# Windowed attention ahead of an expert layer: value matmuls with V as the loaded operand, x turned back together with the gate weights, row sums on ScalarE

## The chip, the cores and the metric
One Trainium2 chip, one NeuronCore. The metric is the device time of one execution in microseconds (us), as the median of several executions. Engines: PE is TensorE (PEld its weight loads), DVE is VectorE, ACT is ScalarE, POOL is GpSimd, SP is SyncE, which here only issues DMAs ("SPq").

## The reference
Three layers follow each other, in float32.

```
scores = (q @ k.T) / sqrt(64); keep keys 0..3 (sinks) and the last 128 up to the query
a = softmax(scores);  x = a @ v                     # 2 batches x 8 heads, 768 x 64
x -> (1536, 512);  logits = x @ w_gate + log1p(exp(x @ w_noise)) * noise
top-2 of 8 experts;  x = sum_k weight_k * relu(x @ w1[e_k]) @ w2[e_k]
h = x @ w_in;  out = (h * tanh(softplus(h))) @ w_out
```

## The kernel before, in words
The program is one core's, with every engine's order of work written out by hand and semaphores between them. Four stages follow: attention (to about 123 us), routing (to about 143 us), 31 expert slots of 128 rows, and the last layer.

**Attention.** The 16 heads make 8 head pairs. A head pair has 6 query tiles of 128 rows, so there are 48 tiles ("units" u). The loops of PE, ACT and DVE take two tiles at a time, 24 double steps, of which the middle ones run in a hardware loop (`stream_loop`). A query tile sees its own 128 keys, the 128 keys before and 4 sink keys. For one tile:

- PE `scores` (L1172): 2 heads x 3 split-precision matmuls, 64 rows each, up to 264 columns, into one of two pairs of PSUM banks. It waits until the exponentials of tile u-2 are done.
- DVE `merge_step` (L841): a predicated copy puts the previous tile's masked scores over the own tile's, then L860 takes the row minimum (the scores are negated) for the exponent's bias. The first tile of a head pair masks against a constant; the second also hides the sinks twice seen.
- ACT `exp_step` (L653): one exponential for each head into `probs` (2 buffers).
- PE `turn_probs` (L1199): two transposes of 128 x 128 and one of 8 sink columns. ACT `pT_step` (L662) copies them to SBUF, the sinks by an instruction of their own (L668).
- POOL `cut_probs` (L539): two selects separate the probabilities of own and previous keys.
- PE `values` (L1217): the probabilities are the loaded operand (128 columns) and V streams, 130 columns for own and previous keys, 162 for the sinks. A float32 matmul is two passes, each a weight load and a stream. V carries a column of ones, so the sum of the row comes out beside the product, and 16 columns of V times the gate and noise weights, so the logits come out too.
- DVE `norm_step` (L870): the reciprocal of the sum, then one multiply from PSUM into `x_sb`.

V times the gate weights is made by PE `gate_parts` (L1186) from a turned copy of V (`v_turn`, 404.5 KB a head pair): three steps of two tiles each, in the later tiles of the head pair before, copied next to V by ACT `gate_step` (L670).

q and k of the next head pair are rounded by ACT (`round_qk`, L648, four pieces: two in the first double step of a head pair, two in the second) and their remainders taken by DVE (`qk_remainder`, L862). The first of these waits for both loads.

**SP's queue** sets when things are loaded and stored (L432). For head pairs i from 2 to 7, in order:

```
sp.wait_ge(qk_ready, 4 * (i - 1)); load_qk(i)
sp.wait_ge(gates_made, ...);       load_turned(i)
sp.wait_ge(pv_ready, QT * (i - 1)); load_v(i)
store_x(i - 2)       # first: sp.wait_ge(x_ready, QT * (i - 1))
two 512 KB blocks of the first expert's weights (i = 2 to 5)
if i == 4: seven 256 KB stores that fill y_dram
```

POOL's `first_set` (L526) rounds and splits those blocks in the second half of the attention stage, from tile 14 on. After the last tile, DVE `gate_sums` (L894) adds the 8 parts of each logit; the routing follows from there.

Of the kernel before, what the change touches and what calls it, by code (L numbers as in the profile page):

```python
# [4 lines left out]
P = 128  # L5
# [9 lines left out]
def stream_loop(eng, count, body):  # L15

    body(0)
    with eng.Fori(1, count - 1) as i:
        body(i)
    body(count - 1)  # L20


# [11 lines left out]
def attention_moe_mish(nc, shape, q, k, v, v_sinks, v_turned, noise, w1, w2, w_in, w_out, out, n_sink, window):  # L34
# [4 lines left out]
    i32 = mybir.dt.int32  # L39
# [20 lines left out]
    VW = D + 1 + GL  # L60
    SEC = P + NS
    SK = 2 * NS + 1
# [47 lines left out]
    v_in = [attn.tensor(f"v_in{i}", [P, QT, 2, VW], fp32) for i in range(2)]  # L110
    v_sink = [attn.tensor(f"v_sink{i}", [P, 2, VW], fp32) for i in range(2)]
    VT_GATE, VT_TILES, VT_SINK = 0, 2 * GL, 2 * GL + S
    WIDE = 2 * (D + 1)
    v_turn = attn.tensor("v_turn", [P, S + SK + 2 * GL], fp32)
    qT = [attn.tensor(f"qT{i}", [P, 2, S], f32r) for i in range(2)]
    kT = [attn.tensor(f"kT{i}", [P, 2, QT * SEC], f32r) for i in range(2)]
    probs = [attn.tensor(f"probs{i}", [P, 2 * SEC], fp32) for i in range(2)]
    pT = [attn.tensor(f"pT{i}", [P, 2, P], fp32) for i in range(2)]
    pT_own = [attn.tensor(f"pT_own{i}", [P, 2, P], fp32) for i in range(3)]
    pT_prev = [attn.tensor(f"pT_prev{i}", [P, 2, P], fp32) for i in range(3)]  # L120
    pT_sink = [attn.tensor(f"pT_sink{i}", [P, P], fp32) for i in range(3)]
# [8 lines left out]
    x_sb = route.tensor("x_sb", [P, QT, NP, 2, VW], fp32)  # L130
    later = route.tensor("later", [P, P], fp32)
# [9 lines left out]
    ramp_i = route.tensor("ramp_i", [P, P], i32)  # L141
    rt = {}
    for name, cols in (("nb", 4), ("rc", 4), ("seg", E * QT), ("seg_e", E * QT), ("noise", E * NT), ("lgs", GL * NT),
                       ("enx", E * NT), ("sp", E * NT), ("lg", E * NT), ("eq", E * QT), ("cum", E * QT), ("cut", E * QT),
                       ("oh", 2 * E * NT), ("m1", NT), ("m2", NT), ("gap", NT), ("s1", NT), ("c", E * NT), ("inc", E * NT),
                       ("pos", E * NT), ("up", E), ("ns", E), ("incn", E), ("excn", E), ("sel", 2 * E * NT),
                       ("p01", 2 * NT), ("den", NT), ("tab", 32 * E), ("ex", 32)):
        rt[name] = route.tensor("rt_" + name, [P, cols], fp32)
    tok_i = route.tensor("tok_i", [P, 2 * NT], i32)
# [78 lines left out]
    with ctx:  # L228
# [11 lines left out]
        v_turn_loaded = sem("v_turn_loaded")  # L240
# [26 lines left out]
        pT_sink_ready = sem("pT_sink_ready")  # L267
        WEIGHTS_FROM = 14
        pT_cut = sem("pT_cut")
        pv_ready = sem("pv_ready")  # L270
        x_ready = sem("x_ready")
        dve_step = sem("dve_step")
        units_begun = sem("units_begun")

        gates_made = sem("gates_made")
        gates_ready = sem("gates_ready")
# [68 lines left out]
        OB = [bank[6], bank[7]]  # L345
        OUT_HEAD = 256

        def out_heads(b):

            return OB[b].rearrange("p (h d) -> p h d", h=2)[:, :, 0:VW]  # L350

# [17 lines left out]
        GATE_TILES = 2  # L369
        GATE_STEPS = QT // GATE_TILES  # L370
        GATE_AT = QT - GATE_STEPS
        GATE_FIRST = [TP[1][:, n * P:(n + 1) * P] for n in range(GATE_STEPS)]
        GATE_OUT = [TP[0][:, 3 * P:4 * P], TP[1][:, 3 * P:4 * P]]
# [6 lines left out]
        def at_unit(it, n):  # L380

            return it + n // QT // 2, n // QT % 2, n % QT

        MERGES = [0]
        for t in range(QT):
            MERGES.append(MERGES[t] + 1 + (t == 1) + (t > 0 and window < P))
        PER_PAIR = MERGES[QT]

# [13 lines left out]
        def _(sp):  # L402
# [4 lines left out]
            def load_v(i, par):  # L407
                if i < 2:
                    sp.wait_ge(sinks_cleared, i + 1)
                sp.dma_start(v_in[par][:, :, :, 0:D + 1], v[i]).then_inc(v_loaded[par], 16)  # L410
                sp.dma_start(v_sink[par][0:SK, :, 0:D + 1], v_sinks[i]).then_inc(v_loaded[par], 16)

            def load_turned(i):
                sp.dma_start(v_turn[:], v_turned[i]).then_inc(v_turn_loaded, 16)
# [9 lines left out]
            load_turned(0)  # L424
# [3 lines left out]
            sp.wait_ge(gates_made, GATE_STEPS)  # L428
            load_turned(1)
            sp.dma_start(rt["noise"][:].rearrange("p (j e) -> p j e", j=NT), noise.rearrange("(j p) e -> p j e", p=P)).then_inc(route_in_loaded, 16)  # L430
            assert UNITS <= 2 * (NP - 2)
            for i in range(2, NP):  # L432
                sp.wait_ge(qk_ready, 4 * (i - 1))
                load_qk(i, i % 2)
                sp.wait_ge(gates_made, GATE_STEPS * i)
                load_turned(i)
# [8 lines left out]
                if i == 4:  # L445
# [31 lines left out]
        def _(pool):  # L477
# [17 lines left out]
            for i in range(3):  # L495
                nc.gpsimd.memset(pT_sink[i][:], 1.0)
# [15 lines left out]
            nc.gpsimd.iota(ramp_i[:], pattern=[[1, P]], base=0, channel_multiplier=0)  # L512
# [8 lines left out]
            nc.gpsimd.tensor_copy(ramp[:], ramp_i[:])  # L521
# [17 lines left out]
            def cut_probs(u):  # L539
                b = u % 3  # L540
                pool.wait_ge(pT_ready, u + 1)
                wait(pool, pv_ready, u - 2)
                ins = nc.gpsimd.affine_select(out=pT_own[b][:], in_=pT[u % 2][:], compare_op=ALU.is_ge, fill=0.0, base=0,  # L543
                                              pattern=[[0, 2], [1, P]], channel_multiplier=-1)
                if u % QT > 0:
                    ins = nc.gpsimd.affine_select(out=pT_prev[b][:], in_=pT[u % 2][:], compare_op=ALU.is_ge, fill=0.0, base=-1,
# [3 lines left out]
            for n in range(0, NP * QT, 2):  # L550
                cut_probs(n)
                cut_probs(n + 1)
# [90 lines left out]
        def _(act):  # L643
# [9 lines left out]
            def exp_step(hp, par, t):  # L653
                u, b = QT * (2 * hp + par) + t, t % 2
                act.wait_ge(bias_ready, u + 1)
                wait(act, probs_transposed, u - 1)
                for hd in range(2):
                    ins = nc.scalar.activation(probs[b][:, hd * SEC:(hd + 1) * SEC], SC[b][:, hd, SEC:2 * SEC], ACT.Exp,  # L658
                                               bias=rt["nb"][:, 2 * b + hd:2 * b + hd + 1], scale=-1.0)
                ins.then_inc(probs_ready, 1)  # L660

            def pT_step(hp, par, t):  # L662
                u, b = QT * (2 * hp + par) + t, t % 2
                act.wait_ge(probs_transposed, u + 1)
                wait(act, pT_cut, u - 1)
                nc.scalar.activation(pT[b][:], TP[b][:, 0:2 * P].rearrange("p (h q) -> p h q", h=2), ACT.Copy).then_inc(pT_ready, 1)  # L666
                wait(act, pv_ready, u - 2)
                nc.scalar.activation(pT_sink[t % 3][0:2 * NS, :], TP[b][0:2 * NS, 2 * P:3 * P], ACT.Copy).then_inc(pT_sink_ready, 1)  # L668

            def gate_step(hp, par, step, src):  # L670
                i = 2 * hp + par
                act.wait_ge(gates_made, GATE_STEPS if isinstance(hp, int) and i == 0 else GATE_STEPS * i + step + 1)
                if step == 0:
                    wait(act, pv_ready, QT * (i - 1))
                at = slice(GATE_TILES * step, GATE_TILES * (step + 1))
                ins = nc.scalar.activation(v_in[par][:, at, :, D + 1:VW],
                                           src[:, 0:GATE_TILES * 2 * GL].rearrange("p (t h e) -> p t h e", t=GATE_TILES, h=2), ACT.Copy)
                if step == GATE_STEPS - 1:
# [801 lines left out]
```

## Time and profile before

| What | us |
|---|---|
| median of 3 runs (lowest, highest) | 805.99 (805.07, 806.14) |
| the profiled execution, its own time | 804.93 |
| its span on the core | 803.2 |
| PE, PEld, DVE, ACT, POOL busy | 775.8, 643.2, 517.0, 278.8, 304.0 |

In the profile times count from the start of the span. A busy time of PE is not PE at its peak, since the ends of matmuls are modelled and overlap; the distance between the starts of two instructions tells the pace. A row of the timeline gives start, duration, engine, line, operation, output and inputs, shape, how many instructions were merged into it and, in brackets, how long the engine was idle before it and for whom.

### The profile page before, as it was taken

The numbers are of one execution on the slowest core, as the hardware profiler recorded it, in microseconds if no ns is written. First come the engines' busy times: TensorE is split into PE (matmuls) and PEld (weight loads), VectorE is DVE, ScalarE is ACT, GpSimd is POOL, SyncE is SP. The second block draws the span as 40 slices with busy tenths as digits, with TensorE's granted clock in tenths as the row PEclk, the third lists the DMA queues.
The fourth block names the chain that finished last, engine by engine and source line by source line (L and its number), as shares of the span: only waits on it lengthen the run. The fifth ranks groups of instructions, "written<-read, shape, count | busy, mean of one in ns | idle before, by whom it ended". The sixth has DMA issues, their size and how long they took to land.

```text
span 803.2 us, 13152 instructions
## 1 busy us (share of the span) xinstructions
PE 775.8 (97%) x4116; PEld 643.2 (80%) x4117; DVE 517.0 (64%) x944; ACT 278.8 (35%) x553; POOL 304.0 (38%) x307
## 2 busy tenths in 40 slices
PE   9999994999999999999999999998999999999997
PEld 6888883788888888888888888786888888888886
DVE  5686876454454454454544544558998888888776
ACT  5665652203110302003030300145555555454453
POOL 3366672929281652817337554550111010000000
PEclk9999996999999999999999999999999999999999
DMA  7689562736372451715427353120100100000001
GB/s 204 184 237 304 146 207 55 208 103 199 104 223 79 125 175 37 228 62 156 144 62 227 102 184 109 37 66 1 53 27 27 53 27 27 1 28 25 1 0 53
DMA packets 61442, 86.15 MB, mean 107 GB/s; under 512 B 30104, under 2 KB 34200, under 8 KB 61400
## 3 DMA queue, kind: packets, MB, share of 16 engines
q1 hardware_dynamic: 43400, 37.23, 15.1%
q10 hardware_dynamic: 13600, 33.96, 14.1%
q0 software_dynamic: 4400, 14.42, 6.4%
q8 instruction: 23, 0.38, 0.2%
q14 instruction: 19, 0.16, 0.1%
HBM read 69.35 MB, written 16.25 MB: 107 GB/s over the span
## 4 chain that ended last, share of the span: by engine, by line
PE 88%; DVE 5%; ACT 2%; SPq 1%; issue 1%; DMA 1%; another core or an unknown queue 1%; POOL 0%; DVEq 0%; ACTq 0%; POOLq 0%
PE bank L1321 21%; PE bank L1332 21%; PE bank L1393 15%; PE bank L1374 15%; PE bank L1229 4%; PE bank L1305 3%; PE bank L1182 2%; PE bank L1298 2%; PE bank L1192 1%; PE bank L1214 1%; PE bank L1232 1%; SPq L448 1%; PE bank L1167 1%; DMA k_in<-in_k 1%
## 5 line engine op out<-in xcount | busy, mean ns | idle before, releaser
L563 POOL TENSOR_TENSOR wgt<-stage,wgt 128x1024 f32 (+1 forms) x64 | 151.2, 2403 | 106.6 <-ACT wgt L738 106.6
L1332 PE MATMUL bank<-wgt,hT 128*128 (+1 forms) x744 | 185.7, 398 | 0.0
L1321 PE MATMUL bank<-wgt,xT 128*128 (+1 forms) x744 | 182.4, 394 | 1.5 <-DVE xT L1049 1.5
L1321 PEld LDWEIGHTS bank<-wgt,xT 128*128 128x128 f32 x744 | 137.3, 188 | 28.9 <-DVE xT L1049 1.7
L1332 PEld LDWEIGHTS bank<-wgt,hT 128*128 128x128 f32 x744 | 135.2, 188 | 25.8
L738 ACT ACTIVATE wgt<-stage 128x1024 f32 (+1 forms) x64 | 61.6, 1045 | 269.6 <-PE bank L1332 259.4
L1393 PE MATMUL bank<-wgt,gT 128*128 128x512 f32 x576 | 141.2, 395 | 4.9 <-DVE gT L1110 4.9
L1374 PE MATMUL bank<-x2T,wgt 128*128 128x512 f32 (+1 forms) x588 | 138.1, 385 | 0.9 <-DVE x2T L1087 0.9
L1393 PEld LDWEIGHTS bank<-wgt,gT 128*128 128x128 f32 x576 | 108.5, 190 | 28.6 <-DVE gT L1110 6.1
L1374 PEld LDWEIGHTS bank<-x2T,wgt 128*128 128x128 f32 x588 | 108.7, 188 | 23.0 <-POOL wgt L635 1.1
L1055 DVE TENSOR_SCALAR h<-bank 128x512 f32<-128x512 f32 x62 | 42.9, 691 | 63.9 <-PE bank L1321 61.8
L1059 DVE CAST hT<-bank 128x512 fp32r<-128x512 f32 x62 | 42.9, 692 | 58.3 <-PE bank L1305 58.3
L808 ACT ACTIVATE recd<-nume,ones 128x512 f32<-128x512 f32 x48 | 34.8, 725 | 90.8 <-DVE nume L1133 90.8
L1070 DVE COPY y_sb<-bank 128x512 f32<-128x512 f32 x31 | 21.4, 692 | 69.5 <-PE bank L1332 55.9
L609 POOL DMA_INDIRECT ya<-y_dram,y_idx x10 | 10.2, 1019 | 132.0 <-PE bank L1366 114.9
L1061 DVE TENSOR_TENSOR hT<-bank,hT 128x512 fp32r<-128x512 f32 x62 | 42.9, 692 | 2.1
L1124 DVE TENSOR_SCALAR expv<-expv 128x512 f32<-128x512 f32 x48 | 20.7, 431 | 32.4 <-ACT expv L802 32.4
L795 ACT ACTIVATE gT<-nume 128x512 fp32r<-128x512 f32 x48 | 30.3, 632 | 28.0 <-DVE nume L1101 27.7
L543 POOL TENSOR_SCALAR_AFFINE_SELECT pT_own<-pT 128x256 f32<-128x256 f32 x48 | 20.9, 436 | 48.6 <-ACT pT L666 48.1
L1305 PEld LDWEIGHTS bank<-ident,h 128*128 128x128 f32 x248 | 30.6, 140 | 9.5 <-DVE h L1055 1.6
L1305 PE MATMUL bank<-ident,h 128*128 128x128 f32 x248 | 37.3, 273 | 0.5 <-DVE h L1055 0.4
L658 ACT ACTIVATE probs<-bank,rt_nb 128x132 f32<-128x132 f32 x96 | 30.1, 366 | 21.8 <-DVE rt_nb L860 21.6
(169 smaller groups left out, 963.7 us busy)
## 6 DMA issues: line engine op xcount, KB each, us to landing
stage<-in_moe_w ACTq DMA_DIRECT2D x48, 512.0 KB, 4.3
stage<-in_moe_w SPq DMA_DIRECT2D x16, 512.0 KB, 6.7
y_dram<-y_sb SPq DMA_DIRECT2D x31, 256.0 KB, 2.4
stage<-in_moe_w_in ACTq DMA_DIRECT2D x8, 512.0 KB, 4.5
stage<-in_moe_w_out ACTq DMA_DIRECT2D x8, 512.0 KB, 3.7
v_turn<-in_v_turned SPq DMA_DIRECT2D x8, 404.5 KB, 3.7
v_in<-in_v SPq DMA_DIRECT2D x8, 390.0 KB
x_dram<-x_sb SPq DMA_DIRECT2D x16, 192.0 KB, 3.2
```

Of the source, the lines that this page charges most:

```text
L563: nc.gpsimd.tensor_tensor(cols(parity, 1, u * UNIT, UNIT), stage[:, u, :], cols(parity, 0, u * UNIT, UNIT).bitcast(fp32), ALU.subtract).th ...
L738: nc.scalar.activation(cols(parity, 0, u * UNIT, UNIT), stage[:, u, :], ACT.Copy).then_inc(rounded, 1)
L808: nc.scalar.activation(recd[p][:], nume[p][:], ACT.Ln, bias=ones1[:, 1:2]).then_inc(ln_ready, 1)
L1055: V.tensor_scalar(h[:, half * 512:(half + 1) * 512], bank[half][:], 0.0, None, ALU.max).then_inc(h_ready, 1)
L1059: V.tensor_copy(hT[:, 0, 4 * half:4 * half + 4], src).then_inc(hT_rounded, 1)
L1061: V.tensor_tensor(hT[:, 1, 4 * half:4 * half + 4], src, hT[:, 0, 4 * half:4 * half + 4].bitcast(fp32), ALU.subtract).then_inc(hT_ready, 1)
L1229: T.matmul(OB[b][:, to:to + WIDE], (pT_prev if back else pT_own)[t % 3][:, hd, :], v_in[par][:, t - back].rearrange("p h d -> p (h d)")[:, ...
L1305: ins = T.transpose(bank[3 + half][:, n * P:(n + 1) * P], h[:, c * P:(c + 1) * P], ident[:])
L1321: ins = T.matmul(HA[half][:], xT[:, a, c, :], cols(par, b, c * F + half * 512, 512), start=c == 0 and n == 0, stop=c == NC - 1 and n == 2)
L1332: ins = T.matmul(YB[kk % 2][:], hT[:, a, c, :], cols(par, b, NC * UNIT + c * DM, DM), start=c == 0 and n == 0, stop=c == F // P - 1 and n ...
L1374: ins = T.matmul(hid_bank(fg)[:, tok], wgt[:, 0, b, c * F2 + f * P:c * F2 + (f + 1) * P], x2T[g % 2][:, a, c, tok], start=c == 0 and n == ...
L1393: ins = T.matmul(bank[s][:], gT[fg % 2][:, a, s * P:(s + 1) * P], wgt[:, 1, b, f * DM:(f + 1) * DM], start=f == 0 and n == 0, stop=f == NF ...
```

## The change
The value matmul is turned round: halves of V (128 keys x 64 columns, one for each head) are loaded and the turned probabilities stream, so that x comes out turned, head 0 in output partitions 0 to 63 and head 1 in 64 to 127. ACT copies it to SBUF (`copy_xT`), and a matmul with `turn_back` (an identity beside the gate weights) gives x with its logit parts. The sinks go through the same copies as the other keys. The row sums come from the exponentials' accumulator output; POOL adds 1e-9 and DVE takes one reciprocal for two tiles. Row minima, x copy and norm are one instruction for two tiles. `probs`, `pT`, `pT_own` and `pT_prev` have 4 buffers. The steps of a tile are spread over more double steps: scores in step u, turned in u+2, values in u+4, turned back and normed in u+6. `v_turn`, `gate_parts` and `gate_step` go. The loops are unrolled. The fill of y_dram moves from i == 4 to i == 7. The diff's core:

```diff
-                sp.dma_start(v_in[par][:, :, :, 0:D + 1], v[i]).then_inc(v_loaded[par], 16)
+                sp.dma_start(v_in[par][:], v[i]).then_inc(v_loaded[par], 16)
...
             for i in range(2, NP):
                 sp.wait_ge(qk_ready, 4 * (i - 1))
                 load_qk(i, i % 2)
-                sp.wait_ge(gates_made, GATE_STEPS * i)
-                load_turned(i)
                 sp.wait_ge(pv_ready, QT * (i - 1))
                 load_v(i, i % 2)
                 store_x(i - 2)
...
-                if i == 4:
+                if i == NP - 1:
                     sp.wait_ge(consts_ready, 1)
...
+            def pad_sums(u):
+                nc.gpsimd.tensor_scalar(scale_cols("rs", u, 2), scale_cols("rs", u, 2), 1.0e-9, 1.0, ALU.add,
+                                        ALU.mult).then_inc(sums_padded, 2)
+            for n in range(0, PROBS + 2, 2):
+                if n > 0:
+                    cut_probs(n - 2)
+                    cut_probs(n - 1)
+                    pad_sums(n - 2)
...
+            def exp_step(u):
+                b, m = u % 2, u % 4
                 act.wait_ge(bias_ready, u + 1)
+                wait(act, probs_transposed, u - 3)
                 for hd in range(2):
+                    ins = nc.scalar.activation(probs[m][:, hd * SEC:(hd + 1) * SEC], SC[b][:, hd, SEC:2 * SEC], ACT.Exp,
+                                               bias=rt["nb"][:, 2 * b + hd:2 * b + hd + 1], scale=-1.0,
+                                               accum_out=scale_cols("rs", u, 1)[:, hd:hd + 1])
                 ins.then_inc(probs_ready, 1)
+            def pT_step(u):
                 act.wait_ge(probs_transposed, u + 1)
+                wait(act, pv_ready, u - 3)
+                nc.scalar.activation(pT[u % 4][:], TP[u % 2][:, 0:3 * P].rearrange("p (h q) -> p h q", h=3), ACT.Copy).then_inc(pT_ready, 1)
+            def copy_xT(u, count):
+                to = xT_att[u // 2 % 2]
+                act.wait_ge(pv_ready, u + count)
+                wait(act, x_turned, u // 2 * 2 - 2)
+                nc.scalar.activation(to[:, u % 2:u % 2 + count], turned_out(u, count), ACT.Copy).then_inc(xT_copied, count)
...
+            for u in range(0, PROBS, 2):
+                i, t = at_unit(u)
+                if u > 0:
+                    pT_step(u - 2)
+                    pT_step(u - 1)
+                exp_step(u)
+                exp_step(u + 1)
+                if u >= 4:
+                    copy_xT(u - 4, 2)
+                if i + 1 < NP and t < 4:
+                    par1 = (i + 1) % 2
+                    if t == 0:
+                        wait(act, scores_ready, QT * i)
+                        act.wait_ge(q_loaded[par1], 16 * ((i + 1) // 2 + par1))
+                        act.wait_ge(k_loaded[par1], 16 * ((i + 1) // 2 + par1))
+                    round_qk(par1, t)
+                    round_qk(par1, t + 1)
...
+            def row_minima(u, count):
+                b = u % 2
+                dve.wait_ge(merged, merges[0])
+                V.tensor_reduce(rt["nb"][:, 2 * b:2 * (b + count)], banks[:, 2 * b:2 * (b + count), SEC:2 * SEC], AX.X,
+                                ALU.min).then_inc(bias_ready, count)
+            def norm_step(u, count):
+                i, t = at_unit(u)
+                dve.wait_ge(scales_ready, u + count)
+                dve.wait_ge(x_turned, u + count)
+                scales = scale_cols("rs", u, count).rearrange("p (b h) -> p b h", h=2).unsqueeze(3)
+                V.tensor_tensor(x_sb[:, t:t + count, i], back_out(u, count), scales.broadcast_to([P, count, 2, VW]),
+                                ALU.mult).then_inc(x_ready, count)
...
+            for u in range(0, PROBS, 2):
+                i, t = at_unit(u)
+                merge(u)
...
+                merge(u + 1)
...
+                    row_minima(u, 2)
+                if u >= 4:
+                    row_scales(u - 4)
+                if t > 0 and i + 1 < NP:
+                    qk_remainder(i + 1, t - 2)
+                    qk_remainder(i + 1, t - 1)
+                if u >= 6:
+                    norm_step(u - 6, 2)
...
+            def values(u):
+                i, t = at_unit(u)
+                par, m, to = i % 2, u % 4, turned_out(u, 1)[:, 0]
...
+                wait(pe, xT_copied, u // 2 * 2)
                 pe.wait_ge(pT_cut, u + 1)
+                parts = [(v_in[par][:, t], pT_own[m][:, 0], pT_own[m][:, 1])]
+                if t > 0:
+                    parts.append((v_in[par][:, t - 1], pT_prev[m][:, 0], pT_prev[m][:, 1]))
+                parts.append((v_sink[par], pT[m][:, 2], pT[m][:, 2]))
+                for n, (keys, *of) in enumerate(parts):
                     for hd in range(2):
+                        ins = T.matmul(to[hd * D:(hd + 1) * D], keys[:, hd], of[hd], start=n == 0, stop=n == len(parts) - 1)
+                ins.then_inc(pv_ready, 1)
+            def turn_x_back(u):
...
+                pe.wait_ge(xT_copied, u + 1)
+                wait(pe, x_ready, u // 2 * 2)
+                T.matmul(back_out(u, 1)[:, 0], xT_att[u // 2 % 2][:, u % 2], turn_back[:, u // QT % PPB], start=True, stop=True).then_inc(x_turned, 1)
+            for u in range(0, PROBS, 2):
+                scores(u)
+                scores(u + 1)
+                if u == 0:
+                    fill(2)
+                else:
+                    turn_probs(u - 2)
+                    turn_probs(u - 1)
+                if u == 2:
+                    fill(1)
+                if u >= 6:
+                    turn_x_back(u - 6)
+                    turn_x_back(u - 5)
+                if u >= 4:
+                    values(u - 4)
+                    values(u - 3)
+            turn_probs(PROBS - 2)
+            turn_probs(PROBS - 1)
+            for u in (PROBS - 6, PROBS - 4):
+                turn_x_back(u)
+                turn_x_back(u + 1)
+                values(u + 2)
+                values(u + 3)
+            turn_x_back(PROBS - 2)
+            turn_x_back(PROBS - 1)
```

## Rows read from the trace of the kernel before

**Rows 1.** Timeline of PE in the attention stage: starts of the score blocks, two tiles each.

```profile
6.11 0.97 PE L1182 MATMUL bank<-kT,qT 64*128 64x132 f32 x12
...
34.34 0.97 PE L1182 MATMUL bank<-kT,qT 64*128 64x132 f32 x12
...
38.45 1.00 PE L1182 MATMUL bank<-kT,qT 64*128 64x264 f32 x12
...
42.69 0.99 PE L1182 MATMUL bank<-kT,qT 64*128 64x264 f32 x12
...
48.00 0.97 PE L1182 MATMUL bank<-kT,qT 64*128 64x132 f32 x12
...
113.77 0.99 PE L1182 MATMUL bank<-kT,qT 64*128 64x264 f32 x12
```

**Rows 2.** Timeline of PE, the rest of the double step that starts at 38.45.

```profile
39.38 0.71 PE L1229 MATMUL bank<-v_in,pT_own 128*128 128x130 f32 x4
39.93 0.44 PE L1232 MATMUL bank<-v_sink,pT_sink 128*128 128x162 f32 x2
40.20 0.61 PE L1229 MATMUL bank<-v_in,pT_own 128*128 128x130 f32 x4
...
41.09 0.44 PE L1232 MATMUL bank<-v_sink,pT_sink 128*128 128x162 f32 x2
41.37 0.38 PE L1214 MATMUL bank<-ident,probs 128*128 128x128 f32 x2
41.59 0.27 PE L1215 MATMUL bank<-ident,probs 128*8 128x128 f32 x1
```

**Rows 3.** Timeline of DVE at the end of the stage: the two gate sums.

```profile
121.07 1.24 DVE L898 TENSOR_REDUCE rt_lgs<-x_sb 128x80 f32<-128x640 f32 x1
...
122.78 0.37 DVE L898 TENSOR_REDUCE rt_lgs<-x_sb 128x16 f32<-128x128 f32 x1
```

**Rows 4.** Timeline of DVE in the double step of 38.45.

```profile
39.26 0.43 DVE L850 COPY_PREDICATED bank<-later,bank 128x256 f32<-128x256 uint32 x1 [0.73 <-PE bank L1182]
...
40.52 0.43 DVE L860 TENSOR_REDUCE rt_nb<-bank 128x2 f32<-128x264 f32 x1
...
41.42 0.55 DVE L868 SCALAR_TENSOR_TENSOR qT<-q_in,qT 128x384 fp32r<-128x384 f32 x1
...
42.19 0.33 DVE L878 TENSOR_TENSOR x_sb<-bank,rt_rc 128x162 f32 x1
```

**Rows 5.** ACT: timeline of the same step, then its shortest group by form.

```profile
40.19 0.63 ACT L658 ACTIVATE probs<-bank,rt_nb 128x132 f32<-128x132 f32 x2 [0.19 <-DVE rt_nb L860]
...
41.90 0.39 ACT L666 ACTIVATE pT<-bank 128x256 f32<-128x256 f32 x1 [0.28 <-PE bank L1215]
...
L679 ACT ACTIVATE v_sink<-bank 9x32 f32<-9x32 f32 x8 | 1.4, 172 | 0.0
```

**Rows 6.** Timeline of SP's queue: one pass with expert blocks, the y fill, one without.

```profile
25.77 1.04 SPq L420 DMA_DIRECT2D x_dram<-x_sb  x2
...
28.88 0.43 SPq L405 DMA_DIRECT2D k_in<-in_k  x1
...
55.63 7.68 SPq L448 DMA_DIRECT2D y_dram<-ident  x7
...
82.50 1.04 SPq L420 DMA_DIRECT2D x_dram<-x_sb  x2
...
84.22 0.55 SPq L405 DMA_DIRECT2D k_in<-in_k  x1
```

**Rows 7.** The k loads' time from issue to landing, and ACT's wait after the y fill.

```profile
DMA to landing us min/median/max: 4.5/5.9/7.3
...
69.09 0.52 ACT L650 ACTIVATE qT<-q_in 128x384 fp32r<-128x384 f32 x1 [2.14 <-DMA k_in<-in_k]
```

**Rows 8.** PE gap and clock: busy PE, PEld, DVE, ACT, POOL by stretch, PEclk, DMA share, GB/s.

```profile
543.60:547.80 4.20, 0.35 (x2) 0.00 (x0) 2.62 (x5) 2.46 (x4) 0.00 (x0) 1.00 0.01 2
547.90:551.30 3.40, 3.40 (x8) 2.74 (x9) 3.31 (x5) 2.60 (x5) 0.00 (x0) 0.50 0.00 0
```

More of the change, by code:

```diff
@@ L378, in of_group, with at_unit @@
             return rt[name][:, g * IN_GROUP:(g + 1) * IN_GROUP]
[L380 to L387, printed above, removed]
+        def at_unit(u):
+            return u // QT, u % QT
         FIRST = 3
@@ L839, in heads, with merge @@
                 return a.unsqueeze(1).broadcast_to([P, 2, a.shape[1]])
-            def merge_step(hp, par, t):
-                u, b = QT * (2 * hp + par) + t, t % 2
+            merges = [0]
+            def merge(u):
+                b, t = u % 2, u % QT
                 dve.wait_ge(scores_ready, u + 1)
@@ L870, in norm_step @@
[L870 to L879 removed]
+                    merges[0] += 1
@@ L1232, in values @@
-                T.matmul(out_heads(b), pT_sink[t % 3][:], v_sink[par][:],
-                         start=False, stop=True).then_inc(pv_ready, 1)
-            def body(it):
-                last = isinstance(it, int) and it == NP // 2 - 1
-                first = isinstance(it, int) and it == 0
-                for n in range(0, 2 * QT, 2):
-                    hp, par, t = at_unit(it, n)
-                    final = last and n == 2 * QT - 2
-                    scores(hp, par, t)
-                    scores(hp, par, t + 1)
-                    if first and n == 0:
-                        for step in range(GATE_STEPS):
-                            gate_parts(0, step, GATE_FIRST[step])
-                    else:
-                        if first and n == 2:
-                            fill(1)
-                        values(*at_unit(it, n - 2))
-                        if not final:
-                            values(*at_unit(it, n - 1))
-                    turn_probs(hp, par, t)
-                    if first and n == 0:
-                        fill(1)
-                    if final:
-                        values(*at_unit(it, n - 1))
-                    turn_probs(hp, par, t + 1)
@@ L1448 @@
     vt = inputs["v"].reshape(pairs, 2, tiles, P, dim)
[L1449 to L1452 removed]
+    laid["v"] = vt.transpose(0, 3, 2, 1, 4)
+    held = _np.zeros((pairs, 2 * sinks, 2, dim), _np.float32)
     for h in range(2):
[L1454 to L1467 removed]
+        held[:, h * sinks:(h + 1) * sinks, h] = vt[:, h, 0, 0:sinks]
     laid["v_sinks"] = held
+    both = _np.concatenate([inputs["moe_w_gate"], inputs["moe_w_noise"]], axis=1)
+    laid["gates"] = both.reshape(heads // 2, 2 * dim, -1).transpose(1, 0, 2)
     arrays, args = {}, []
```

345 lines of the change are left out of this document (114 added, 231 removed).

## The prediction, made before the changed kernel ran

> **What bounds the kernel now.** I read four views in this order: the starts of the score matmuls, which mark the steps of the attention stage; one step on each engine; SP's own queue; the clock. The attention stage takes 24 double steps, each two query tiles of one head pair; call them D0 to D23, so that head pair i has D(3i), D(3i+1) and D(3i+2). They start at 6.11, ..., 34.34 (D6), 38.45 (D7), 42.69 (D8), 48.00 (D9), ..., 113.77 (D23) [rows 1]. One double step is 4.11 us without gate matmuls; the third of a head pair, with two sets of them, is 5.31; a head pair is 13.66. The steps are full of TensorE work: in D7 the score block takes 0.93 (38.45 to 39.38), the value matmuls 0.45 per four and 0.28 per two sink passes (40.20 to 41.09 to 41.37), a turn of probabilities 0.11 an instruction (two in 0.22) [rows 2]. Sum: 0.93 + 2 x (0.89 + 0.28) + 2 x 0.33 + about 0.2 = 4.1, which is the step. So TensorE bounds this stage. A change of matmul shape costs about 0.1 on each side of the first instruction: the first four value passes take 0.55, the later ones 0.45 [rows 2]; with the gap before them I count 0.2 per change of shape, two changes per double step.
>
> All after the routing (the expert and Mish stages) is untouched by the diff, so the question is when the gate sums of the last tile are ready: 122.78 + 0.37 = 123.15 now [rows 3].
>
> **The change, part by part.**
>
> TensorE. Value matmuls: 8 value and 4 sink passes per tile (12, where 10 were), each with 64 weight columns, the two heads to different halves of the output partitions. A pass streams 128 columns, as the 130 of now, so 0.11 each [rows 2]. In sequence that is 1.31 per tile; with the two heads side by side 0.66. No row shows column halves. What rows show is the nearest case, the scores, where the heads take different row halves: 12 passes of up to 264 columns in a block of 0.93 including both changes of shape, against 12 x 0.11 = 1.3 in sequence [rows 2]. I take 0.66, the row it resembles most, and keep 1.31 as the other end. The page "TensorEngine Tiling (Array Packing)" of the Trainium skill, section "Key Properties", says that tiles work independently and in parallel, and also that a change of tiling mode drains the engine; by the first the sum stays as I have it, by the second alone it gains one more change of shape per double step, which the next sentence counts from rows anyway. Double step: scores 0.72 (0.93 less 0.2), turns 0.66, turning x back 4 passes of 160 columns, the 0.14 of the 162-column sink passes [rows 2], 0.55, values 1.32, three changes of shape 0.6: 3.85 (3.6 where one of the two tiles is the first of its sequence). The gate matmuls go.
>
> The new chain inside a step. Both tiles now share one row-minimum instruction, after both merges. From the start: the merge begins at +0.81 (39.26), 0.43; the second ends at +1.65; the reduction of 528 columns: 0.43 for 264 [rows 4] plus 264 x about 1.04 ns = 0.71, to +2.4; four exponentials, two take 0.63 with a pitch of 0.27 [rows 5]. The row sums add an accumulator read after each. No row has it: below 0, above 0.17, the smallest ScalarE instruction [rows 5]; I take 0.1, since short instructions overlap here. The last exponential ends at +4.05, and the second tile's scores of the next step may start 0.36 after the first's: a step of 3.7 to 3.85, in the first step of a head pair 4.05 (longer merge, sink merge). So TensorE and this chain tie near 3.9, against 13.66 / 3 = 4.55 now. VectorE: 2.0 for merges, minima and reciprocal, at most 1.1 for two remainders (0.55 each), 0.5 for the norm (0.33 for 162 columns, 320 now) [rows 4]. ScalarE: two wider copies 0.8 (0.39 for 256 columns [rows 5]), exponentials 1.5, copy of x 0.3, rounding 0.9: 3.5. POOL: four cuts of 0.41 and up to 1.8 of weight rounding, 3.5, and has a step of slack. All just below 3.9. The gate copies and the sink copy on ScalarE go; they were hidden by TensorE, so worth nothing alone.
>
> SP's queue, where I expect the change to be decided. SP does for each i: load q, k of head pair i; wait for the values of pair i-2; load v; **wait for x of pair i-2**, store it; load two expert blocks (i = 2 to 5); then load q, k of i+1. Now x of pair i-2 is normalised in D(3i-3); k is issued 3.1 after the store (25.77 to 28.88) [rows 6], lands 4.5 / 5.9 / 7.3 (lowest, median, highest) later [rows 7], and ScalarE needs it late in D(3i). Delaying that by the 7.68 of y fill stores cost one wait of 2.14 [rows 6, 7], so the slack is 5 us. With the deeper pipeline the same x is normalised in the third step of its successor pair: norm(u-6) stands at the end of step u. For pair 0 that is D5 instead of D3, and k of pair 3 is still needed in D6. Chain from the start of D5: merges, minima, reciprocal and two remainders to +4.1, norm to +4.7 (with the second score block 0.2 later after a stall, and some POOL contention); 0.1 + 3.1 + 5.9 to the landing of k, +13.8; then ScalarE: two roundings 0.95, two copies 0.8, two exponentials 0.84, 0.1 of semaphores = 2.7, then D8's scores may start: +16.5. ScalarE's order puts the copies and exponentials of D7 behind the wait for k, so all three engines stand behind it; TensorE is idle for about 5 us.
>
> The clock. From 543.6 to 547.8 TensorE was busy for 0.35 of 4.20 us, and from 547.9 to 551.3 it was granted 0.50, the lower level [rows 8]. I expect the same after gaps of 5 us; as the chain, not TensorE, then sets the time, it costs the longer scores and turns in D8: 0.4 to 0.8. I add 0.5: a period of 17.0 per head pair, against 11.65 without the wait.
>
> The sum, on the clock of the trace: D0 6.1; it needs no gate work, 3.1; D1 to D5 take 3.85 + 3.75 + 4.05 + 3.85: D5 at 24.7. Four periods of 17.0 (k of pairs 3 to 6): D17 at 92.7. For pair 7 no expert blocks stand ahead: k issues 1.7 after the store (82.50 to 84.22) [rows 6] and lands 4.5 later: 4.7 + 0.1 + 6.2 + 2.7 = 13.7, D20 at 106.4. Then 3.75 + 4.05 + 3.85: D23 at 118.1 (113.77 now). The tail is longer, since turning, cutting, values, copy, turn back and norm of the last four tiles follow each other: last exponential +4.1, turn +4.75, values of tiles 44 and 45 to +6.7, copy +7.3, back +7.9, values of 46 and 47 to +9.4, copy and back to +10.1, norm 0.35, gate sums 1.24, norm and last sums 0.7: +12.4 instead of +9.4 [rows 3]. Gate sums at 130.5, 7.3 later than 123.15. The y fill moves to a place where nothing waits for it: its 2.14 is inside the terms above. The profiled execution took 804.93 (span 803.2, 1.7 around it) and the median is 805.99; I add 7.3 to the median: **813**.
>
> **The rivals.**
> 1. Forecast, chance 0.62: the late store holds up the q, k loads; 813, own range 807 to 820 (landing 4.5 to 7.3 gives -5.6 and +5.6, the clock -2 to +2).
> 2. The heads do not run side by side, 0.12. Steps are 5.2 and 4.7. Where the load chain binds (D5 to D17) nothing changes but the clock stays up (-2). Elsewhere: D1 to D4 take 5.2 + 4.7 + 5.2 + 5.2 = 20.3 for 15.5, +4.8; D17 to D20 15.1 for 13.7, +1.4; D20 to D23 15.1 for 11.65, +3.5; tail +1.3; together +9: **822**.
> 3. Short transfers, 0.18. k lands 4.5 after its issue, since v is no longer ahead of it in the queues: 1.4 less per period, 5.6 in all, and with no fall of the clock 2 more: 805.7; with a smaller accumulator price a little under. Speaks for it: less traffic beside it (the v load comes a step earlier, the turned v is gone). Against: the expert blocks are still ahead.
> 4. The loads come in time, 0.08: the other side. ScalarE would find k if it landed within 3.5 us of x's norm; below that every step is 3.9. D5 at 24.7, then 3.75 + 5 x 11.65 + 7.9 gives D23 at 94.6, gate sums at 107.0, 16.2 earlier: **790**. Only the issue of stores and blocks is already 3.1, so this needs a reading error of mine about the order of SP's waits.
>
> **How the numbers follow.** A measurement of this kernel tells about 0.2% (1.6 us) from nothing. Faster: rival 4 and half of rival 3, 0.18. Same: the rest of rival 3 and the edge of the forecast, 0.14. Slower: 0.68. The range 799 to 824 leaves out rival 4 and the top of rival 2, and takes in the bounds of the landing and of the accumulator (0 to 0.17 a piece, 4 a step over some 12 free steps, +-4).
>
> **What would show it.** Right: ScalarE's q rounding waits 4 to 6 us for the k load in the first step of head pairs 2 to 5 and 1 to 2 in pair 6; scores at a distance of 16 to 17.5 per pair there and near 11.7 in pair 1; half clock after each gap; x stores issued about two double steps later than now; value passes starting in pairs. Wrong: no DMA wait ahead of the rounding, or value passes 0.11 apart in one row (rival 2), or free steps above 4.3.

## The result and the profile after

The changed kernel takes 812.74 us (median, 810.64 to 813.45) against 805.56 (805.07 to 806.14) for the kernel before on the same chip: a ratio of 1.0085, 95% interval 1.0064 to 1.0105. It is slower by 7 us; 813 was forecast. The profiled execution took 813.45 with a span of 811.7 (before: 804.93 and 803.2). All times below are in us; a time with a plus sign counts from the start of the step named.

The timeline of PE gives the starts of the score blocks, the counterpart of [rows 1]: D5, D6, D7, D8, D9, D11, D14, D17, D20 and D23.

```profile
25.48 1.00 PE L1177 MATMUL bank<-kT,qT 64*128 64x264 f32 x12
29.00 1.16 PE L1177 MATMUL bank<-kT,qT 64*128 64x132 f32 x12
32.90 1.31 PE L1177 MATMUL bank<-kT,qT 64*128 64x264 f32 x12
41.17 1.73 PE L1177 MATMUL bank<-kT,qT 64*128 64x264 f32 x12 [4.15 <-ACT probs L657]
46.22 0.97 PE L1177 MATMUL bank<-kT,qT 64*128 64x132 f32 x12
...
57.56 1.73 PE L1177 MATMUL bank<-kT,qT 64*128 64x264 f32 x12 [2.49 <-ACT probs L657]
74.09 1.41 PE L1177 MATMUL bank<-kT,qT 64*128 64x264 f32 x12 [2.40 <-ACT probs L657]
90.56 1.35 PE L1177 MATMUL bank<-kT,qT 64*128 64x264 f32 x12 [2.91 <-ACT probs L657]
104.78 0.99 PE L1177 MATMUL bank<-kT,qT 64*128 64x264 f32 x12
117.47 0.76 PE L1177 MATMUL bank<-kT,qT 64*128 64x264 f32 x8
```

From D1 to the start of D7 the steps are 3.5 to 4.1 long, shorter than before. Then TensorE stands idle ahead of D8, D11, D14 and D17, and from D5 on a head pair takes 15.7, 16.4, 16.5, 16.5, 14.2 and 12.7 instead of 13.66. What it waits for stands in ACT's timeline: the rounding of q sits behind the load of k, and the exponentials behind the rounding.

```profile
38.71 0.52 ACT L649 ACTIVATE qT<-q_in 128x384 fp32r<-128x384 f32 x1 [5.01 <-DMA k_in<-in_k]
...
40.30 0.37 ACT L657 ACTIVATE probs<-bank,rt_nb 128x132 f32<-128x132 f32 x1
40.56 0.21 ACT L657 ACTIVATION_READ_ACCUMULATOR probs<-bank,rt_nb 128x1 f32 x1
40.65 0.38 ACT L657 ACTIVATE probs<-bank,rt_nb 128x132 f32<-128x132 f32 x1
```

The waits of the first 140 us (us in total, times, longest) have it four times (5.0, 3.4, 3.3 and 3.8):

```profile
ACT qT L649 <- DMA k_in<-in_k: 15.4, 4, 5.0
```

The load is late because of what stands ahead of it in SP's queue. Its timeline, against [rows 6]:

```profile
29.55 0.97 SPq L410 DMA_DIRECT2D x_dram<-x_sb  x2
30.56 1.15 SPq L432 DMA_DIRECT2D stage<-in_moe_w  x2
31.75 0.44 SPq L397 DMA_DIRECT2D q_in<-in_q  x1
32.24 0.43 SPq L398 DMA_DIRECT2D k_in<-in_k  x1
```

And the landing of the k loads, against [rows 7]:

```profile
DMA to landing us min/median/max: 3.6/6.3/7.2
```

The store was at 25.77 before; although this kernel is ahead in its steps (D6 starts at 29.00, for 34.34 before), it stores x 3.8 later. The gap and the clock behind it, by stretch (length; busy PE, PEld, DVE, ACT, POOL; granted clock, DMA share, GB/s):

```profile
36.75:41.17 4.42, 0.27 (x6) 0.03 (x2) 1.44 (x3) 2.46 (x9) 1.06 (x3) 0.99 0.46 171
41.17:44.60 3.43, 3.43 (x20) 3.20 (x21) 1.85 (x5) 2.44 (x9) 2.88 (x5) 0.51 0.02 5
...
71.42:74.09 2.67, 0.28 (x6) 0.03 (x2) 1.44 (x3) 2.46 (x9) 1.06 (x3) 1.00 0.48 139
74.09:78.00 3.91, 3.83 (x24) 3.09 (x24) 2.66 (x6) 3.24 (x12) 3.67 (x6) 0.64 0.02 6
```

ScalarE is busy only in the last 2.46 of the gap, once it has k; then TensorE is granted 0.51, the lower of its two levels: the six turns of probabilities take 1.54 in D8, 0.87 in D5. The score block takes 1.73 for 1.00, but part of that is the stall and not the clock: in the second experiment below it takes 1.34 behind a wait, at the full clock. The stage ends with the gate sums on DVE, against [rows 3]:

```profile
128.62 1.22 DVE L890 TENSOR_REDUCE rt_lgs<-x_sb 128x80 f32<-128x640 f32 x1
...
130.11 0.37 DVE L890 TENSOR_REDUCE rt_lgs<-x_sb 128x16 f32<-128x128 f32 x1
```

The last one ends at 130.48 (130.11 + 0.37) for 123.15, 7.3 later; the rest of the span is 681.2 for 680.05.

### The profile page after: what moved, and what is told of

Read it like the earlier page. It is cut to its first block, busy times and chain, and to the rows that moved or that the text cites. A ratio compares the mean times of both kernels' runs of the same rounds, so it can differ in the third digit from the quotient of the medians.

```text
span 811.7 us, 13212 instructions
## 1 busy us (share of the span) xinstructions
PE 768.5 (95%) x4198; PEld 631.6 (78%) x4199; DVE 508.9 (63%) x874; ACT 285.6 (35%) x594; POOL 314.4 (39%) x331
## 3 DMA queue, kind: packets, MB, share of 16 engines
q10 hardware_dynamic: 13600, 33.96, 12.7%
## 4 chain that ended last, share of the span: by engine, by line
PE 84%; DVE 6%; ACT 3%; DMA 3%; issue 3%; SPq 1%; POOL 0%; ACTq 0%; DVEq 0%; POOLq 0%
PE bank L1297 21%; PE bank L1308 21%; PE bank L1369 15%; PE bank L1350 15%; PE bank L1281 3%; DMA k_in<-in_k 2%; PE bank L1202 2%; PE bank L1274 2%; PE bank L1177 2%; ACT probs L657 2%; PE bank L1186 1%; PE bank L1211 1%; DVE bank L834 1%; PE bank L1161 1%; PE bank L1342 0%
## 5 line engine op out<-in xcount | busy, mean ns | idle before, releaser
L1177 PE MATMUL bank<-kT,qT 64*128 64x264 f32 (+2 forms) x288 | 28.8, 315 | 18.0 <-ACT probs L657 17.1
L1177 PEld LDWEIGHTS bank<-kT,qT 64*128 64x128 f32 x288 | 20.9, 193 | 28.0 <-ACT probs L657 21.6
L536 POOL TENSOR_SCALAR_AFFINE_SELECT pT_own<-pT 128x256 f32<-128x256 f32 x48 | 22.9, 484 | 40.2 <-ACT pT L665 40.1
L657 ACT ACTIVATE probs<-bank,rt_nb 128x132 f32<-128x132 f32 x96 | 34.3, 373 | 11.4 <-DVE rt_nb L851 11.0
```

The source lines that it names most:

```text
L657: ins = nc.scalar.activation(probs[m][:, hd * SEC:(hd + 1) * SEC], SC[b][:, hd, SEC:2 * SEC], ACT.Exp, bias=rt["nb"][:, 2 * b + hd:2 * b + ...
L1177: ins = T.matmul(SC[b][:, hd, w], qT[par][d, a, t * P:(t + 1) * P], kT[par][d, b2, keys], start=n == 0, stop=n == 2)
```

## Experiments

Theory: the new arithmetic is faster, and the late store of x in SP's queue, ahead of the loads of q and k, gives back more than that. Rivals: the arithmetic itself is slow (heads not side by side, the softmax chain), or the y fill's new place is at fault. "Gate sums at" gives the end of the last gate sum, the end of the stage. Each ratio is to the kernel before as it ran beside that experiment (its medians were 807.4 to 808.6), with its 95% interval; the quotient of the two medians differs from it by up to 0.2%.

**The load ahead of the store.** In the changed kernel:

```diff
+sp.wait_ge(qk_ready, 4); load_qk(2, 0)
 for i in range(2, NP):
-    sp.wait_ge(qk_ready, 4 * (i - 1)); load_qk(i, i % 2)
     sp.wait_ge(pv_ready, QT * (i - 1)); load_v(i, i % 2)
+    if i + 1 < NP:
+        sp.wait_ge(qk_ready, 4 * i); load_qk(i + 1, (i + 1) % 2)
     store_x(i - 2)
```

> The changed kernel with SP's order alone altered: q and k of head pair i+1 are issued ahead of the wait for x of pair i-2, its store and the expert blocks. Theory A (the late store holds the loads up): no k wait ahead of the rounding, double steps of 3.9 throughout, last score block near 96 instead of 117.5, 21 us off: 790 to 793. Rival B (the longer chain of minima, exponentials with their sums and the copy makes the long periods, or the loads are slow by themselves): within 3 us of 812.7.

Measured: 793.68, ratio 0.9812 [0.9778, 0.9846], span 792.2. No engine waits for a load of k, D5 is at 25.72 and D8 at 37.18, gate sums at 110.86. That is just above the 790 to 793 of theory A and far from rival B. One move in SP's queue is worth 19.6 us of the stage, and turns slower into faster. In the stretches from D5 to D8 and from D8 to D11 the steps are full of TensorE work, and the clock stays up:

```profile
25.72:37.18 11.46, 11.39 (x136) 9.68 (x134) 8.51 (x21) 9.73 (x38) 6.22 (x15) 1.00 0.75 233
37.18:48.64 11.46, 11.40 (x136) 9.69 (x134) 8.87 (x20) 9.74 (x38) 10.83 (x18) 1.00 0.74 232
```

**Only the expert blocks behind the load.** The store stays ahead; the two expert blocks of a pass go behind the next q, k load.

```diff
     load_qk(i, i % 2)
+    for u in range(2 * (i - 3), min(2 * (i - 2), UNITS)) if i > 2 else ():
+        src, to = unit_of(0, u); sp.dma_start(to, src).then_inc(unit_loaded[u], 16)
     ...
     store_x(i - 2)
-    for u in range(2 * (i - 2), min(2 * (i - 1), UNITS)): ...
```

> The changed kernel; the store of x stays ahead of the next q and k loads, with its wait, but the two expert blocks go behind them. Theory A with the issue and traffic of the blocks as a part of the chain: periods as the one without blocks in the changed kernel, 14.2 instead of 16.3, four of them, 8 us off: 803 to 806. If only the wait for x counted and not what is issued after it: 810 to 813. Rival B: 812.

Measured: 798.26, ratio 0.9877 [0.9847, 0.9908]; better than the 803 to 806 expected. A head pair takes about 12.9, gate sums come at 115.56. SP's timeline in this kernel:

```profile
29.24 0.97 SPq L410 DMA_DIRECT2D x_dram<-x_sb  x2
30.25 0.59 SPq L397 DMA_DIRECT2D q_in<-in_q  x1
30.89 0.53 SPq L398 DMA_DIRECT2D k_in<-in_k  x1
```

And the landing of its k loads:

```profile
DMA to landing us min/median/max: 3.8/4.4/7.3
```

Behind the store k is issued 1.65 later instead of 2.69, and the median landing falls from 6.3 to 4.4, since 1 MB of weights is no longer ahead of it. So of the 19.6 us, 14.9 go with the blocks and 4.7 with the store. That split holds in this order only: behind the early store of the kernel before, the blocks made no load late. Per head pair the two savings are 1.04 and 1.9, and TensorE's clock stays up on top (ScalarE still waits 8.1 for k in six waits, at most 2.0 at once). The lateness of the store alone would have left the kernel faster than before.

**The late store in the kernel before.** Two edits there: `store_x` waits for four tiles more, `sp.wait_ge(x_ready, min(QT * (i + 1) + 4, QT * NP))`, and the y fill stands at `i == NP - 1`.

> The kernel before with the fill late and the store of x waiting for 4 more tiles, that is about as long as the pipeline of the changed kernel makes it wait. Theory A: k of pairs 3 to 6 lands 13 us after the start of the third double step and is wanted at 10: four waits of about 3, of which 2.6 show: 10 us over the kernel with the fill late alone, 813 to 816. Rival B (the order in SP's queue is no matter in itself): within 2 us of that kernel.

**The y fill alone.** In the kernel before, `if i == 4:` becomes `if i == NP - 1:`.

> The kernel before, with the fill of y_dram moved from i == 4 to i == 7 as the change has it, nothing else. The fill's 7.7 us in SP's queue made one k wait of 2.14 and one double step 1.6 longer: 1.5 us off, 804. If the fill's place is worth nothing: 805.6.

Measured: 821.26, ratio 1.0156 [1.0123, 1.0188], and 805.22, ratio 0.9965 [0.995, 0.998]. The first is the late store with the late fill, the second the fill alone. The y fill's move is a small gain (gate sums at 121.70 for 123.15), not the fault. The late store, with the old arithmetic, puts the gate sums at 137.48, 15.8 later. Its waits show the same signature:

```profile
ACT qT L650 <- DMA k_in<-in_k: 12.9, 4, 4.1
```

The store goes out at 33.86, 8.1 after its place before (3.8 in the changed kernel). The waits are the four of about 3 that were expected, and yet the run took 821 and not 813 to 816. Against the kernel with the fill alone, the four steps that wait for k (D7, D10, D13 and D16) are 3.6, 2.2, 3.2 and 2.7 longer, 11.7 together for the 10 expected. The steps behind three of them are longer too, by 1.6, 1.4 and 0.7. For these the expectation had no term: they carry gate matmuls and are full of TensorE work, and TensorE runs them in part at the lower level (a granted clock of 0.56 from 46.87 to 50.27 and 0.55 from 64.71 to 68.11).

**The kernel before with its loads first**, and the y fill late: the same queue order as in the first experiment.

> The kernel before, with SP's order of the other study kernels: q and k of the next head pair issued as soon as their buffers are free, in front of the store of x and the expert blocks, and the y fill at the end. No load is late then in either kernel, so this against the changed kernel with the loads first (about 793) is what the new arithmetic is worth by itself. Forecast: the kernel before has its loads in time anyway but for the one wait of 2.14 behind the y fill, so as with the y fill alone moved: 804 to 806, score blocks of the head pairs 13.7 apart. Rival: its loads are later than I read from the waits, and more than the y fill's share comes back: under 803.

Measured: 805.29, ratio 0.9962 [0.9949, 0.9975], as with the y fill alone. Beyond the fill's place, queue order is worth nothing there. The ratio of the two kernels with loads first is 0.9812 / 0.9962 = 0.985: the new arithmetic by itself is worth 1.5%, about 12 us; the two ran in different groups of runs, and with both intervals it is 1.1% to 1.9%. The stage alone is 10.6 shorter (gate sums at 110.86 for 121.48).

**What bounds a step once no load is late.** Four edits to the kernel with the loads first. The row sums left out (`accum_out` removed from the exponential, the sums a constant 8, so this kernel leaves out the normalisation of x):

> The kernel with the loads first, whose exponentials give no row sums (the row sums are a constant 8, so x is not normalised; this part of the computation is left out). It asks what bounds a step of about 4.0 once no load is late. Theory A, the chain merge, minima, four exponentials bounds it as nearly as TensorE: each accumulator read adds 0.08 to 0.09 to the pitch of an exponential (0.35 for 0.27), 0.35 per double step, so the steps become 0.2 to 0.35 shorter, the gate sums come 4 to 7 us earlier, 787 to 790. Theory B, TensorE alone bounds it (it is busy 3.5 to 4.0 of every step): only the gaps in front of the second score block shrink, 0 to 2 us, 792 to 794. The accumulator reads of 0.2 vanish from the trace and the pitch of exponentials is 0.27 in both.

The row minima apart:

```diff
 merge(u)
+row_minima(u, 1)
 merge(u + 1)
-row_minima(u, 2)
+row_minima(u + 1, 1)
```

> The kernel with the loads first, with a row-minimum instruction per tile behind its own merge, in place of one for both. Two of 264 columns (0.43 each) for one of 528 (0.71): 0.15 more of VectorE, but the first two exponentials start about 0.9 earlier and the last one ends about 0.6 earlier. Theory A (the chain bounds the step with TensorE): steps 0.2 to 0.5 shorter, 4 to 9 us in all, 785 to 790. Theory B (TensorE bounds): only the steps in which TensorE is idle (0.71 + 0.17 in the third step of three head pairs, and the last, uncovered step) gain, 1 to 3 us, 791 to 793.

Measured: 792.49, ratio 0.9822 [0.9783, 0.9862], without the sums and 791.34, ratio 0.9795 [0.9761, 0.9829], with the minima apart. Both are within 2.4 us of the kernel with the loads first, which these intervals can't tell from nothing, and as theory B has it: TensorE bounds most steps, and the chain through ScalarE holds few of them. With the minima apart TensorE is full to 34.72 of 35 us (25 to 60), and less so later, where POOL and VectorE are as busy:

```profile
25.00:60.00 35.00, 34.72 (x416) 29.93 (x417) 31.22 (x73) 29.91 (x115) 29.71 (x52) 1.00 0.79 238
60.00:95.00 35.00, 32.83 (x388) 27.49 (x387) 32.91 (x74) 26.85 (x107) 33.16 (x57) 1.00 0.63 182
```

The heads one after the other:

```diff
-for n, (keys, *of) in enumerate(parts):
-    for hd in range(2):
+for hd in range(2):
+    for n, (keys, *of) in enumerate(parts):
```

> The kernel with the loads first, with the value matmuls in the order of head 0 (all three products), then head 1, in place of the heads in turn: the same 24 passes per double step, but neighbours now go to the same half of the output columns for 6 passes (12 rows of the trace) at a time. If passes run side by side only with a neighbour of the other half, they start 0.11 apart: the block of 24 takes 2.6 for 1.46, each step is 1.1 longer where TensorE bounds it. Theory B (TensorE alone bounds): 20 to 24 us more, 813 to 818. Theory A (tied with the chain of the softmax, which has 0.2 to 0.5 of slack against TensorE at most): 15 to 20 more. Rival: the engine reorders or overlaps the two heads all the same and nothing changes, 793 to 795.

Measured: 795.68, ratio 0.9847 [0.9812, 0.9883], with gate sums at 112.18 for 110.86. My 813 to 818 was wrong, and the rival was right. In PE's timeline of this kernel (L1205) the second head's first pass (47.99) starts beside the third of the first head (47.98), and from there passes start about 0.055 apart, in an order that isn't the program's:

```profile
47.71 0.43 PE L1205 MATMUL bank<-pT_own,v_in 128*64 128x128 f32 x2
47.98 0.27 PE L1205 MATMUL bank<-pT_prev,v_in 128*64 128x128 f32 x1
47.99 0.32 PE L1205 MATMUL bank<-pT_own,v_in 128*64 128x128 f32 x1
48.09 0.27 PE L1205 MATMUL bank<-pT_prev,v_in 128*64 128x128 f32 x1
48.15 0.27 PE L1205 MATMUL bank<-pT_own,v_in 128*64 128x128 f32 x1
...
49.13 0.38 PE L1205 MATMUL bank<-pT,v_sink 128*64 128x128 f32 x2
49.44 0.99 PE L1180 MATMUL bank<-kT,qT 64*128 64x264 f32 x12
```

Only the first two and the last two passes of a block (the x2 rows) have no partner; the block takes 1.73 instead of 1.46. So here six passes of one half could stand ahead of the six of the other, and all but four of the 24 still ran side by side: the order within a block matters little.

POOL's rounding of a block in two halves:

```diff
-nc.gpsimd.tensor_copy(hi, src).then_inc(rounded_first, 1)
+nc.gpsimd.tensor_copy(hi[:, 0:UNIT // 2], src[:, 0:UNIT // 2])
+nc.gpsimd.tensor_copy(hi[:, UNIT // 2:UNIT], src[:, UNIT // 2:UNIT]).then_inc(rounded_first, 1)
```

> The kernel with the loads first, with POOL's rounding of an expert weight block (1024 columns, 1.04) in two instructions of 512. In the third step of three head pairs VectorE's masking of 8 sink columns takes 1.05, 0.94 and 0.68 in place of 0.17, and the first two end when that POOL instruction ends. Theory: VectorE waits inside its instruction for the POOL instruction to end; with halves (0.52 each) no masking of 8 columns is longer than about 0.75 (the 0.68 that stands beside POOL's cuts stays), and the step with 4.73 becomes 4.3. Rival: the length has nothing to do with the cast (accumulator bank traffic), it stays at 1.05 and 0.94. In all -1 to 0 us, 792 to 794, which one look cannot tell from none; the rows can.

Measured: 794.16 in a single run, too few to tell it from the kernel with the loads first; the rows tell more. What asked for it was this pair in the kernel with the loads first. DVE's timeline has a masking of eight sink columns that takes 1.05, 0.17 elsewhere:

```profile
54.12 1.05 DVE L842 COPY_PREDICATED bank<-later,far 128x8 f32<-128x8 uint32 x1
```

and POOL's timeline the rounding beside it:

```profile
54.10 1.04 POOL L527 CAST wgt<-stage 128x1024 fp32r<-128x1024 f32 x1
```

They end at 55.17 and 55.14. With halves the one that meets a cast is 0.62 (78.77 to 79.39, the cast 78.76 to 79.37); but one met POOL's other rounding instruction and still took 0.95, to 92.87, where that POOL instruction (91.57, 1.28 long) ended, so my bound of 0.75 failed. A third started in the same moment as a cast (both at 54.48) and kept its 0.17. So VectorE is held by a POOL instruction of either kind that is already under way; halving one kind only moves the meeting.

**POOL's last three blocks behind the attention stage.** On top of the minima apart, the condition in the loop becomes `< UNITS - 3`, and the three blocks follow the copy of the ramps.

> The kernel with the loads first and the minima apart, and POOL's rounding of the last three of the eight expert weight blocks (3.6 us each) moved from the attention steps to behind its last instruction before the experts, where it idles for 16.65 us. In the second half of the attention stage (60 to 95 us) TensorE is busy for 32.8 of 35, POOL for 33.2 and VectorE for 32.9, and the last two head pairs take 12.2 and 12.7 for 11.0 to 11.6 before them. Theory P, POOL holds those steps up (with VectorE waiting inside its small instructions for POOL's): the last two head pairs fall to 11.1 to 11.6, the gate sums come 1.5 to 2.5 us earlier, and as the routing that follows has POOL's 10.8 us beside it, it gives back 0 to 1.5 of that: 788.5 to 791. Theory V, VectorE's own work (remainders, x, the routing of the first gate group) holds them up: no change of the steps, the routing 0 to 1.5 later, 791 to 793.

Measured: 792.67, ratio 0.9814 [0.9793, 0.9835], outside the 788.5 to 791 of theory P. Half of that theory held. The last two head pairs fall from 12.2 and 12.7 to 11.7 and 11.4, the gate sums are at 105.25 for 107.43, and TensorE is full in the second half (34.62 of 35). But from there to the first gather on POOL it now takes 18.8 for 13.7. All of it lies in VectorE's chain from the first row below to the `rt_pos` that ends it (8.24 for 3.16 from start to start). DVE's timeline in the routing, the kernel with the minima apart first:

```profile
108.35 0.21 DVE L902 TENSOR_TENSOR rt_lg<-rt_cut,rt_lgs 128x48 f32<-128x48 f32 x1
108.59 0.20 DVE L907 TENSOR_REDUCE rt_m<-rt_lg 128x6 f32<-128x48 f32 x1
108.83 0.21 DVE L908 TENSOR_TENSOR rt_eq<-rt_lg,rt_m 128x48 f32<-128x48 f32 x1
109.07 0.26 DVE L912 TENSOR_TENSOR_SCAN rt_cum<-rt_seg_e,rt_eq 128x48 f32<-128x48 f32 x1
```

and with POOL at work beside it:

```profile
106.17 0.92 DVE L905 TENSOR_TENSOR rt_lg<-rt_cut,rt_lgs 128x48 f32<-128x48 f32 x1
107.12 0.20 DVE L910 TENSOR_REDUCE rt_m<-rt_lg 128x6 f32<-128x48 f32 x1
107.36 1.07 DVE L911 TENSOR_TENSOR rt_eq<-rt_lg,rt_m 128x48 f32<-128x48 f32 x1
108.47 1.24 DVE L915 TENSOR_TENSOR_SCAN rt_cum<-rt_seg_e,rt_eq 128x48 f32<-128x48 f32 x1
```

POOL's timeline beside the latter (x2 is two instructions of 1.24 each):

```profile
105.99 1.04 POOL L527 CAST wgt<-stage 128x1024 fp32r<-128x1024 f32 x1
107.11 2.48 POOL L531 TENSOR_TENSOR wgt<-stage,wgt 128x512 fp32r<-128x512 f32 x2
```

The instructions with two inputs in SBUF take until POOL's current instruction ends, within 0.1; the reduction, with one input, keeps its 0.20 though POOL is busy too. I had priced this at 0 to 1.5; it is 5.1. (2.2 was gained ahead of it, and the rest of the span is 1.7 shorter, which isn't explained.) "SBUF — State Buffer" of the Trainium skill, in its table of terms, says of the port pair that VectorE and GpSimd share that it is locked for a whole instruction and that the loser "fully blocks"; these rows agree.

The best kernel of the study is the changed one with the loads first and the minima apart, 791.34, 2% under the kernel before. Its lead over the one with the loads first alone is within the intervals, so the loads first are what is shown to matter.

## Why the prediction was right, and where its terms were off

The start of every marked step, forecast and measured:

| | D5 | D8 | D11 | D14 | D17 | D20 | D23 | gate sums |
|---|---|---|---|---|---|---|---|---|
| forecast | 24.7 | 41.7 | 58.7 | 75.7 | 92.7 | 106.4 | 118.1 | 130.5 |
| measured | 25.48 | 41.17 | 57.56 | 74.09 | 90.56 | 104.78 | 117.47 | 130.48 |

The mechanism was the forecast one, in its place, and the first experiment and the late store in the old kernel show it from both sides: the wait goes when the load is moved ahead, and comes when the old kernel's store is made late. That the sum agrees to 0.02 is partly luck: the four late periods were 2.9 shorter than forecast, and D5, D20, D23 and the tail together 2.9 longer.

- **The chain of a late period** was forecast at 16.5. For D5 to D8 it is 15.7. x is stored at +4.07 (4.8 forecast): I had allowed for a stall and for POOL. k is issued 2.69 after the store (3.1), because its issue instructions are now shorter than in [rows 6]. ScalarE has k at +13.2, 6.5 after the issue (5.9), and D8's scores start 2.46 later (2.7). ScalarE's waits were 5.0, 3.4, 3.3 and 3.8 for my 4 to 6, and TensorE's idle times 4.2, 2.5, 2.4 and 2.9 for my "about 5": behind the first gap the steps inside a period are longer than I had them (D8 to D10 takes 9.6), but the chain from the store sets the period all the same.
- **The clock** was 0.5 per period. Where the gap came before, x's store is at +4.80 in D8 against +4.07 in D5, so it costs 0.7: the next periods are 16.4 to 16.5. In all four cases the lower level lasts about 3.4, as in [rows 8]: over the 5.0 to 5.5 of the step behind the gap the mean granted clock is 0.67 to 0.69. Without the gaps it does not fall in this stage (the first two experiments). What the fall is worth here without the gap is open; in the late store of the old kernel, whose steps behind the gap are full of TensorE work, it fits the 0.7 to 1.6 by which they grew.
- **Value matmuls side by side**: forecast 0.66 per tile; a row of four passes starts every 0.22, and the block of 24 with its change of shape is 1.46 (31.44 to 32.90). Rival 2 is excluded.
- **The accumulator read** shows as an instruction of 0.21, but the pitch of the exponentials grows from 0.27 to 0.35: 0.08 for my 0.1.
- **The free step**: 3.52 to 4.09 for my 3.75 to 4.05. "TensorE and this chain tie near 3.9" was half right: without the sums the stage gains 3.1 us and with the minima apart 3.4, over some twenty steps, so TensorE is the bound and the chain stands just behind it.
- **D17 to D20** is the step of the prediction that failed: I had a chain of 13.7 through the last k load, with a wait of 1 to 2 for it. There is none: ScalarE gets to the rounding of q only at 101.41, at +10.85, and finds k there, and the 14.2 come from the steps themselves. D17 to D18 takes 5.49 behind the last gap, with 3.4 at the lower clock, and D18 to D19 4.56, in which VectorE's first mask takes 1.41 for 0.43 beside POOL's weight rounding.
- **D20 to D23** took 12.7 for 11.65: I had given VectorE and POOL slack. The experiment on POOL's last blocks shows that its weight rounding lengthens these steps, by 1.25 in the last head pair of the kernel with the minima apart.
- **The tail**: 13.0 for 12.4.
- **Rival 4** put the kernel with loads in time at 790 and D23 at 94.6; it measured 793.7 and 97.85. Of the 3.2 at D23, 1.0 is there at D5; much of the rest is in three steps of 4.7, 4.5 and 5.1, in the first of which the held masking above stands, so POOL's term explains it at least in part. The reading that the order of SP's waits excludes rival 4 was right.
- **Rival 3** asked whether short transfers save the kernel. With v loaded earlier the landing did not shorten (6.3), since the expert blocks were still ahead; with these behind (the second experiment) it did, to 4.4.
- **Behind the stage** the prediction had no term. The rest is 1.2 longer. The first expert matmuls (from 150.3) run at half clock for 3.4 us, which they don't in the kernel before (from 142.8), but the old kernel with its loads first does it too (0.52 from 141.1), so it isn't a property of the change.
- **Slips of arithmetic** that changed nothing: rival 4 and half of rival 3 have a chance of 0.17 and not 0.18, and 7.68 less 2.14 leaves a slack of 5.5 and not 5.

## What to carry to other kernels

When a pipeline is made deeper, look at what a shared queue now waits for: a store that waits for a result two steps later holds every load behind it, and the transfers between the two count twice, in issue time (1.04 here) and in landing time (1.9). Loads whose buffers are free go ahead of stores whose data isn't ready. And idle time on GpSimd is not free for its work while VectorE runs a chain of short two-input instructions.

## What the runs showed of the hardware

- Passes that go to different column halves (128x64 weights, 128 columns streamed) start 0.055 apart, and still do so when the program puts the six passes of one half ahead of the six of the other; I had expected only neighbours to overlap.
- VectorE's short two-input instructions (0.17 to 0.26) stretch to 0.9 to 1.3 beside a POOL instruction of 1.04 to 1.28 that is under way and end with it, within 0.1; a one-input reduction (0.20) beside the same work does not.
- Behind a stretch of 2.67 with 0.28 of TensorE work (71.42 to 74.09) the clock was lower for about 3.4, as behind the longer ones, though not at once: it was 1.00 to 75.00 and 0.53 from there to 78.40.
- With 1 MB of loads ahead in the same queue the median landing of a 396 KB load is 6.3, without them 4.4.
